# Where the first MLP's squares are made: VectorE's multiply or ScalarE's Square, in place

## The reference

```python
def _moe_ref(x, w_in, w_out):      # first MLP
    h = x @ w_in
    r = np.maximum(h, 0.0)
    g = r * r
    return (g @ w_out).astype(np.float32)

def _moe2_ref(x, w_in, w_out):     # second MLP
    h = x @ w_in
    g = h - np.tanh(h)
    return (g @ w_out).astype(np.float32)
```

## Time and profile before

| | |
|---|---|
| median of 3 runs | 877.7 us |
| the profiled execution's own time | 878.23 us |
| its span, first to last instruction | 876.2 us |
| TensorE busy | 866.7 us (99%) |
| VectorE busy | 592.6 us (68%) |
| ScalarE busy | 453.1 us (52%) |
| GpSimd busy | 495.5 us (57%) |
| granted TensorE clock, mean | 0.999 |

### The profile page before, as it was taken

How to read it: one execution, slowest core, us unless ns; L and a number is a source line. 1 busy time by engine, 2 the same in 40 slices (tenths; PEclk the granted TensorE clock), 3 DMA queues, 4 the chain that set the end, 5 groups by cost and what they waited for, 6 DMA issues and landing times.

```text
span 876.2 us, 15491 instructions
## 1 busy us (share of the span) xinstructions
PE 866.7 (99%) x6115; PEld 715.9 (82%) x6115; DVE 592.6 (68%) x813; ACT 453.1 (52%) x860; POOL 495.5 (57%) x377
## 2 busy tenths in 40 slices
PE   8999999999999999999999999999999999999998
PEld 7778888888888888888888888888888888888886
DVE  7886656636654664443465787787787787787775
ACT  7543223222323323221234877777777777777775
POOL 7756634444543634332348676666666666666664
PEclk9999999999999999999999999999999999999999
DMA  7641111303111130202122000000000100000100
GB/s 268 250 142 72 59 60 62 116 1 118 61 59 60 60 116 3 85 34 108 37 73 73 0 1 1 37 1 1 37 1 0 37 1 1 37 1 1 37 1 36
DMA packets 12312, 47.06 MB, mean 54 GB/s; under 512 B 1488, under 2 KB 2384, under 8 KB 12240
## 3 DMA queue, kind: packets, MB, share of 16 engines
q1 hardware_dynamic: 12096, 45.95, 14.7%
q10 hardware_dynamic: 144, 0.13, 0.0%
HBM read 41.36 MB, written 4.72 MB: 53 GB/s over the span
## 4 chain that ended last, share of the span: by engine, by line
PE 93%; DVE 3%; DMA 1%; issue 1%; POOL 1%; ACT 0%; SPq 0%; DVEq 0%; POOLq 0%
PE acc L655 14%; PE acc L656 14%; PE acc L657 14%; PE hid L655 10%; PE hid L656 10%; PE hid L657 10%; PE sc L656 4%; PE sc L657 4%; PE sc L655 4%; PE y L720 2%; PE sc L689 2%; PE y L704 2%; PE sc L742 1%; DVE area L932 1%; DMA x2T<-in_nat 1%
## 5 line engine op out<-in xcount | busy, mean ns | idle before, releaser
L393 POOL TENSOR_TENSOR g_l<-g_f,g_h 128x512 fp32r<-128x512 f32 x96 | 129.3, 1349 | 171.2 <-ACT g_h L496 171.2
L655 PE MATMUL acc<-g_h,wout_h 128*128 128x512 f32 x564 | 222.2, 394 | 0.3 <-DVE area L950 0.3
L656 PE MATMUL acc<-g_l,wout_h 128*128 128x512 f32 x564 | 219.7, 390 | 0.0
L657 PE MATMUL acc<-g_h,wout_l 128*128 128x512 f32 x564 | 219.6, 389 | 0.0
L496 ACT ACTIVATE g_h<-g_f 128x512 fp32r<-128x512 f32 x96 | 60.4, 630 | 272.9 <-DVE g_f L971 272.4
L404 POOL TENSOR_TENSOR area<-area 128x512 f32<-128x512 f32 x96 | 126.2, 1315 | 102.6 <-ACT area L514 102.6
L655 PE MATMUL hid<-x_h,win_h 128*128 128x512 f32 (+1 forms) x435 | 169.0, 388 | 0.0
L656 PE MATMUL hid<-x_l,win_h 128*128 128x512 f32 (+1 forms) x435 | 168.6, 388 | 0.0
L657 PE MATMUL hid<-x_h,win_l 128*128 128x512 f32 (+1 forms) x435 | 168.5, 387 | 0.0
L409 POOL TENSOR_TENSOR g_l<-g_f,g_h 128x512 fp32r<-128x512 f32 x95 | 126.6, 1333 | 31.6 <-ACT g_h L529 31.6
L655 PEld LDWEIGHTS acc<-g_h,wout_h 128*128 128x128 f32 x564 | 105.8, 188 | 24.8 <-issue 1.5
(11 more groups left out here) (145 smaller groups left out, 1151.2 us busy)
## 6 DMA issues: line engine op xcount, KB each, us to landing
x2T<-in_nat SPq DMA_DIRECT2D x10, 736.0 KB, 6.1
area<-in_nat SPq DMA_DIRECT2D x10, 736.0 KB, 5.5
x2T<-in_tt SPq DMA_DIRECT2D x10, 512.0 KB, 4.4
area<-in_tt SPq DMA_DIRECT2D x10, 512.0 KB, 3.6
out<-x2T SPq DMA_DIRECT2D x17, 256.0 KB, 2.0
x2T<-in_win SPq DMA_DIRECT2D x4, 768.0 KB, 7.6
x2T<-in_wout SPq DMA_DIRECT2D x4, 768.0 KB, 6.6
area<-in_win SPq DMA_DIRECT2D x4, 768.0 KB, 4.4
```

Source lines behind the costliest of these rows:

```text
L393: pool.tensor_tensor(g_l[:, m % 4, :], g_f[:, m % 2, :], g_h[:, m % 4, :].bitcast(F32), ALU.subtract).then_inc(s_gl1, 1)
L655: pe.matmul(dst, wh, xh, start=first, stop=False)
L656: pe.matmul(dst, wh, xl, start=False, stop=False)
L657: return pe.matmul(dst, wl, xh, start=False, stop=last)
```

## The change

`act1` on VectorE keeps only the relu. `hi1` on ScalarE first waits for the relu, squares g_f in place with an activation of the kind Square, waits for this, and then rounds as before. The semaphores and their counts stay what they were: s_relu after the relu, s_g1 after the square, s_gh1 after the rounding. Buffers, the order of all other instructions, and TensorE's, GpSimd's and SyncE's programs are the same.

```diff
             def hi1(m):
+                g = g_f[:, m % 2, :]
+                act.wait_ge(s_relu, m + 1)
+                act.activation(g, g, ACT.Square).then_inc(s_g1, 1)
                 act.wait_ge(s_g1, m + 1)
                 after(act, s_o1, m - 3)
                 act.activation(g_h[:, m % 4, :], g_f[:, m % 2, :], ACT.Copy).then_inc(s_gh1, 1)
...
                 dve.tensor_scalar(g, hid1[m % 2], 0.0, None, ALU.max).then_inc(s_relu, 1)
-                dve.wait_ge(s_relu, m + 1)
-                dve.tensor_tensor(g, g, g, ALU.mult).then_inc(s_g1, 1)
```

## The result

Twelve runs of each kernel: 875.88 us with the change (875.5 to 877.95) against 877.78 before (877.03 to 878.75). The ratio is 0.9982 with an interval of 0.9975 to 0.999: about 1.6 us faster, 0.9 to 2.2 by the interval. The medians are 1.90 us apart and the ratio gives 1.58, so it stands at the edge of the 1.75 us under which the prediction counts a difference as "the same".

What follows compares the result with a forecast made beforehand. TensorE was taken as the bound, full from 95 to 477 us, so only four early stalls could change: 0.4 - 0.3 - 0.2 - 0.7 = -0.8 us, from 877.7 to 876.9 us, with an 8-in-10 range of 875.6 to 878.4.

Steps and rivals of the forecast that it cites:

- the early stalls: Four early tiles' keys-values products wait on TensorE for the next tile's mask; 2.27 us in all beyond 2.40 us each.
- the cover: ScalarE's idle time hides the moved squares; without it each step would be 0.66 us longer at most, 63 us over 96.
- The price in the sum: In the full stretch from 95 to 477 us, the squares moved to ScalarE cost no time.
- The square's cost: On ScalarE, 0.63 us per square; about 0.66 us more queue per step, 1.32 us for two ahead of diagonal 5.
- Stall 1: Keys-values product after the scores at 42.76 us: TensorE goes on 0.4 us later; bounds 0.5 earlier, 1.1 later.
- relief (b): Unit 3's transfer, issued after VectorE's subtraction, and ScalarE's work behind it come 0.7 us earlier; bounds 0 and 1.57.
- The distance of 3.7 to 3.9 us: Sign of being right: the product starts this long after the scores at about 42.4 to 42.8, released by ScalarE's diagonal.
- The slower rival: ScalarE's queue bounds the start at diagonal 5, 1.1 us later there; sum +0.8, 878.5 us; chance 0.20.
- Stalls 2, 3 and 4: Products after scores at 59.07, 74.79 and 90.42 us: without VectorE's multiplies they change by -0.3, -0.2 and -0.7 us.
- theory A: Follow-up forecast: the 0.96 us between both kernels' first matmuls into hid is chance, so repeat traces start elsewhere.
- theory B: Follow-up forecast: the change moves the early part, so first matmuls into hid repeat at 22.82 and 21.86 within 0.1.

Runs made afterwards that it cites:

- b2: Against the kernel before, only steps 16 to 95 squared on ScalarE: 877.79 us, ratio 0.9997.
- b4: The changed kernel with every rounding from step 16 on made twice on ScalarE: 878.38 us, ratio 1.0004 to the kernel before.
- a1: The kernel before, run again without edit for a second trace: 878.42 us, ratio 1.0005.
- a3: Against the kernel before, only steps 0 and 1 squared on ScalarE: 876.82 us, ratio 0.9984.
- b3: Against the kernel before, only steps 10 and 13 squared on ScalarE: 877.17 us, ratio 0.9985.
- a2: The changed kernel, run again without edit for a second trace: 876.31 us, ratio 0.9975 to the kernel before.
- c2: The changed kernel, with VectorE's subtraction for unit 3 made to wait for GpSimd's first g_l: 879.79 us, ratio 1.0016 to the kernel before.
- b1: Against the kernel before, all steps but step 1 squared on ScalarE: 878.97 us, ratio 1.0011.

## Why the prediction was right, and where it was not

**The frame held.** TensorE is full behind 95 us, and only the early stalls count: b2 shows it with 80 steps moved for nothing. b4 corrects the reason. I put the cover at ScalarE's idle time, 273 of 382 us; at one place in the last block b4 shows that 0.66 us more in a step is already too much. The price in the sum was 0 and was right, since square and multiply take about the same there.

**The square's cost.** Predicted 0.63 us and 1.32 us for the two ahead of diagonal 5; measured 0.628 and 1.32. No table was loaded.

**Stall 1.** Predicted +0.4, with bounds of -0.5 and +1.1. Counted from the first matmul into hid to the first product, the kernel before has 23.31 and 23.67 us, the changed one 23.09, 23.84 and 23.49. On average nothing (23.49 and 23.47), and -0.6 to +0.5 between single traces. The term of the sum that was mis-sized is relief (b), with "stays blocked by GpSimd as the multiply was": I took 0.7 us, and the load of unit 3 came on average 1.3 us earlier after the first matmul into hid (8.75 and 9.12 us before; 7.25, 8.12 and 7.58 after), which is just the price of the two squares. Whether the subtraction is blocked is a race between two starts 0.1 to 0.6 us apart, and it falls out either way from run to run. The rest of the chain held: in the seven traces with squares 2 and 3 on ScalarE the first product starts 15.7 to 16.0 us after that load, whether the load came at 7.06 or at 9.49 us. I also missed that TensorE's wait before its first product into acc goes with it: from the first matmul into hid it is 10.29 and 10.67 us before, 9.82 to 9.86 in the three traces after. The distance of 3.7 to 3.9 us that I named was nearly met by 3.96, and then missed by 4.65 and 4.33; the scores that I put at 42.4 to 42.8 started at 40.99.

**What the distances hide.** I listed the stalls from the scores to the product, and took the start of the scores as given. It was not: in the kernel before, the mask of tile 4 ended at 41.91 + 0.74 = 42.65 us and the scores of tile 5 began at 42.76. In all five traces with the squares of steps 2 to 4 on VectorE (before, a1, a3, b2, b3) they began 0.10 to 0.12 us after this mask, and the first distance was 3.37 or 3.38 us whenever the load came, since both of its ends stood behind VectorE, with a relu and a multiply between. So relief of VectorE moved the scores too: from the first matmul into hid they began after 19.94 and 20.29 us before, after 19.13 to 19.19 in the three traces of the changed kernel. It did not help there, as ScalarE's diagonal came last for the product.

**The clock.** Not in the prediction at all. After 2.09 and 2.51 us of idle at the first stall the granted clock fell, for 1.6 us (a2, c2). In b1's and b4's profiled runs, with 2.17 and 2.29 us of idle, it stayed at 1.00, but a second stall stood in the same place: from the first product to the second it is 16.64 and 16.24 us there, 16.94 and 16.96 in a2 and c2, and 15.4 where neither happened. The clock alone is therefore not the price, and it is not the change's own: five runs of the kernel before had a mean of 0.998 too (879.15 to 880.55 us), and none of them was profiled. The slower rival, ScalarE's queue, was thus real in b1 and c2: they are slower than the kernel before.

**Stalls 2, 3 and 4.** Predicted -0.3, -0.2 and -0.7; measured -0.37, -0.22 and -0.67. The distances are 2.40 to 2.43 us in nearly all traces with these squares on ScalarE (b1, b4 and c2 have one longer one each, behind a late first product). b3 shows that the third goes with the blocked subtraction (4.02 us before, 3.50 without the multiply); its size is not that alone, for a3 and b2 have 2.55 with the subtraction still at 4.02 and 4.03. Of the fourth it shows that the multiply is not the only cause.

**What is missing from the sum.** -0.8 was predicted, and the first trace has -2.6: -0.96 ahead of the first matmul into hid, -0.22 from there to the first product (predicted +0.4), -1.27 from the first product to the fourth (predicted -1.2), and -0.15 behind it. The first has no term in the sum. There TensorE of the kernel before waits, in the middle of an attention product, for no instruction of another engine:

```profile
20.95 1.07 PE L720 MATMUL acc<-area,x2T 128*32 128x128 f32 x31
22.62 0.27 PE L720 MATMUL acc<-area,x2T 128*32 128x128 f32 x1 [0.60 <-issue]
22.82 0.39 PE L655 MATMUL hid<-x_h,win_h 128*128 128x256 f32 x1
```

The changed kernel's traces have no such gap. I expected chance (theory A), and theory B, 22.82 and 21.86 again within 0.1, is not exact either (22.61, 21.91, 21.58). The five traces with most or all early squares on VectorE (before, a1, a3, b2, b3) have 22.3 to 23.2; eight of the nine with them on ScalarE have 21.3 to 21.9, the ninth, c2, 22.97. So the gap goes with the kernel more than with the run, though no changed instruction had been executed by then. What sets it stays open: no experiment here touched it. It is about half of the 1.8 us between the mean spans of the two kernels' traces (876.3 of two, 874.5 of three); for the runs without a trace it is not on record.

So stalls 2 to 4 were right with their cause, and the rest of the agreement is partly luck. The sum lacks 0.9 us of gain from an early gap, and it lacks the race and what hangs on it, which in part of the runs took up to 2.4 us back (873.6 against 876.0). With these errors of opposite sign the median came 1.0 us under the forecast and 0.3 us inside the range.

## What to carry to other kernels

When one engine is full but for a short start, list its stalls with the distance to a stall-free repetition of the same stretch, and price a change by these alone; three of four were right to 0.1 us here. Count from a point ahead of everything that the change touches as well, for both ends of such a distance can wait for the same engine. Moving work to an idle engine is free only where its queue has no backlog: the version that kept two of the 96 squares where they were gained 3.3 us instead of 2.2, though its trace does not show how much of that the two squares made. Where two engines share a port and their starts lie within some tenths of a microsecond, treat the outcome as open, see what starts each of them, and look at a second trace before explaining the first.

## What the runs showed of the hardware that I had not expected

TensorE went to half its clock after an idle of 2.09 us that followed dense work, for about 3 us (granted clock 0.50 to 0.51, matmuls 0.43 us apart). In c2 it did so after 2.51 us. First stalls of 0.8 to 1.8 us of idle did not do this in these traces, nor did those of 2.17 us (b1) and 2.29 us (b4). "SBUF — State Buffer" of the Trainium skill, section "SBUF: two separate sides", has the first to start keep the port for its whole instruction; the pairs of 1.93 with 2.81 us and of 2.78 with 1.29 us agree.
